# An attention and mixture-of-experts kernel on one core: rows of the negated maxima by VectorE block transposes and ScalarE copies

## What is computed

```python
factor = 2
scale = 1.0 / np.sqrt(D)
q_pool = q.reshape(B, H, S // factor, factor, D).mean(axis=3)
scores = scale * np.matmul(q_pool, k.transpose(0, 1, 3, 2))
scores = scores - np.max(scores, axis=-1, keepdims=True)
attn = np.exp(scores)
attn = attn / (np.sum(attn, axis=-1, keepdims=True) + 1e-09)
return np.matmul(attn, v).astype(np.float32)
```

## Time and profile before

| | us |
|---|---|
| median of 3 runs | 932.74 (932.3 to 933.03) |
| the profiled execution | 933.13 |
| its span, first to last instruction | 931.1 |
| PE busy | 901.1 (97%) |
| DVE busy | 568.9 (61%) |
| ACT busy | 387.7 (42%) |
| POOL busy | 389.2 (42%), all in the attention stage |

### The profile page before, as it was taken

How to read it: one execution, slowest core, us unless ns; L and a number is a source line. 1 busy time by engine, 2 the same in 40 slices (tenths; PEclk the granted TensorE clock), 3 DMA queues, 4 the chain that set the end, 5 groups by cost and what they waited for, 6 DMA issues and landing times.

```text
span 931.1 us, 17697 instructions
## 1 busy us (share of the span) xinstructions
PE 901.1 (97%) x7120; PEld 728.4 (78%) x7120; DVE 568.9 (61%) x966; ACT 387.7 (42%) x740; POOL 389.2 (42%) x269
## 2 busy tenths in 40 slices
PE   4899999999999999999999999999999999999996
PEld 3676766677676766665999999999999999999733
DVE  6988888888888988866554433433443433433423
ACT  3555555565555555555443222322322322322202
POOL 3999999999999989988000000000000000000000
PEclk9999999999999999999999999999999999999999
DMA  6112212222212212303320000200000000377898
GB/s 240 46 59 77 71 36 74 78 78 77 73 57 77 62 43 77 95 1 114 91 91 1 1 1 1 91 1 1 1 1 1 1 1 1 122 239 225 286 382 307
DMA packets 47025, 76.39 MB, mean 82 GB/s; under 512 B 3296, under 2 KB 32608, under 8 KB 46944
## 3 DMA queue, kind: packets, MB, share of 16 engines
q1 hardware_dynamic: 46944, 75.26, 24.2%
HBM read 70.53 MB, written 4.72 MB: 81 GB/s over the span
## 4 chain that ended last, share of the span: by engine, by line
PE 88%; DVE 5%; POOL 2%; DMA 2%; SPq 1%; issue 1%; ACT 1%; POOLq 0%; ACTq 0%
PE psum L611 14%; PE psum L680 8%; PE psum L682 7%; PE psum L664 7%; PE psum L662 7%; PE psum L681 7%; PE psum L663 7%; PE psum L590 6%; PE psum L533 4%; PE psum L593 3%; PE psum L595 3%; PE psum L597 3%; DVE mx L1142 2%; POOL acc L1499 2%; PE psum L493 1%; SPq L469 1%
## 5 line engine op out<-in xcount | busy, mean ns | idle before, releaser
L1499 POOL TENSOR_TENSOR acc<-acc,pt 128x576 f32<-128x576 f32 x220 | 324.1, 1473 | 33.8 <-ACT pt L936 2.8
L936 ACT ACTIVATE pt<-psum 128x576 f32<-128x576 f32 x288 | 174.1, 649 | 121.7 <-PE psum L598 120.6
L1142 DVE TENSOR_REDUCE mx<-psum 128x1 f32<-128x512 f32 x256 | 162.0, 676 | 25.9 <-PE psum L533 25.1
L611 PE MATMUL psum<-pt,vs 128*64 128x288 f32 x1152 | 154.9, 414 | 0.0
L1330 DVE TENSOR_SCALAR gf<-gf 128x384 f32<-128x384 f32 x96 | 34.5, 359 | 196.4 <-ACT gf L1065 196.4
L680 PE MATMUL psum<-gh,W 128*128 128x384 f32 x384 | 133.4, 347 | 0.0
L1065 ACT ACTIVATE gf<-psum 128x384 f32<-128x384 f32 x96 | 47.2, 492 | 200.8 <-PE psum L664 200.2
L681 PE MATMUL psum<-gl,W 128*128 128x384 f32 x384 | 128.5, 335 | 0.0
L682 PE MATMUL psum<-gh,W 128*128 128x384 f32 x384 | 128.4, 334 | 0.0
L664 PE MATMUL psum<-xh,W 128*128 128x384 f32 x384 | 128.4, 334 | 0.0
L662 PE MATMUL psum<-xh,W 128*128 128x384 f32 x384 | 128.4, 334 | 0.0
(11 more groups left out here) (163 smaller groups left out, 1835.5 us busy)
## 6 DMA issues: line engine op xcount, KB each, us to landing
ring<-in_w SPq DMA_DIRECT2D x16, 1024.0 KB, 5.2
ring<-in_w SPq DMA_DIRECT2D x32, 512.0 KB, 7.8
qraw<-in_qT SPq DMA_DIRECT2D x16, 576.0 KB, 4.8
kraw<-in_kT SPq DMA_DIRECT2D x16, 576.0 KB, 3.7
vs<-in_v SPq DMA_DIRECT2D x16, 576.0 KB, 4.0
out<-ob SPq DMA_DIRECT2D x18, 256.0 KB, 4.4
wst<-in_w_in SPq DMA_DIRECT2D x16, 256.0 KB, 2.7
wst<-in_w_out SPq DMA_DIRECT2D x16, 256.0 KB, 3.0
```

Source lines behind the costliest of these rows:

```text
L611: ins = mm(psum[64 * s:64 * s + 64, O_BANK, 0:HALF], vs[:, p % NB, s, kt * D:(kt + 1) * D], pt[:, i % NPT, s, :], start=(kt == 0), stop=(k ...
L936: act.activation(pt[:, i % NPT, :, :], t_pair(("T", h, kt))[:, :, 0:HALF], ACT.Exp, scale=SCALE)\
L1142: dve.tensor_reduce(mx[:, b, u // 2, s, u % 2:u % 2 + 1], bank, AX.X, ALU.max).then_inc(s_red, 1)
L1499: pool.tensor_tensor(a, first, pt[:, i % NPT, :, :], ALU.add).then_inc(s_acc, 1)
```

## The change

PE's transposes of the negated maxima, their three kinds of ring items and ScalarE's copies from PSUM go. `nm2` becomes `nmb` [128, 5 blocks, 2 heads, 32], of which column 0 of each 32 holds the maxima and the rest stays zero, and DVE transposes it in blocks of 32 x 32 to `rows`. There each group of 32 queries (a = 0 to 3 within a block of 128) stands as a row on partition 32a. Copies bring the four partitions' pieces together in `nmT`: one copy for each a and each head, eight a pair, by ScalarE, from one partition to one partition, 5 or 4 blocks of 32 columns each. ScalarE does four after the exponential kt 6 of the odd half and four after kt 8. For pair 0 the first three blocks go by four copies of ScalarE and four of DVE, the others by eight copies of ScalarE after half 0. DVE has three reduces in place of two a pair, then waits for them and transposes. Scores wait for eight copies of a pair. `mx` moves, and the wait for the identity matrix goes to a later user.

```diff
-    r_items = [("S", 0, u) for u in FIRST_UNITS] + [("TRA", 0)]
+    r_items = [("S", 0, u) for u in FIRST_UNITS]
...
-        if h == 0:
-            r_items.append(("TRB", 0))
-        if rows_at(h):
-            r_items.append(("TR", h // 2 + 1))
...
+    def row_to(b, s, a, blocks):
+
+        return nmT[64 * s:64 * s + 1, b, :].rearrange("o (j a c) -> o j a c", a=4, c=32)[:, blocks, a, :]
+
+    def row_from(s, a, blocks):
+        return rows[32 * a:32 * a + 1, blocks, s, :]
+
+    ROW_BLOCKS = (slice(0, 5), slice(0, 5), slice(0, 4), slice(0, 4))
...
-        def max_rows(p):
-            item = ("TR", p)
-            for freed in r_free[item]:
-                pe.wait_ge(*freed)
-            pe.wait_ge(s_nm, 2 * p + 2)
-            lo, hi = r_bank(item, 0), r_bank(item, 1)
-            for j in range(4):
-                nc.tensor.transpose(lo[0:65, j * P:(j + 1) * P], nm2[:, p % 2, j, :], ident[:, :])
-            nc.tensor.transpose(hi[0:65, 0:P], nm2[:, p % 2, 4, :], ident[:, :]).then_inc(s_TR, 1)
...
-                    pe.wait_ge(s_trc, 3 * p + 3)
+                    pe.wait_ge(s_trc, 8 * p + 8)
...
         def read_first_rows():
-            act.wait_ge(s_TRa, 1)
+            act.wait_ge(s_rowsa, 1)
             act.wait_ge(s_zero, 3)
-            act.copy(nmT[0:65, 0, 0:3 * P], r_bank(("TRA", 0))[0:65, 0:3 * P]).then_inc(s_trca, 1)
+            for a in range(4):
+                act.copy(row_to(0, 0, a, slice(0, 3)), row_from(0, a, slice(0, 3))).then_inc(s_trca, 1)
...
-            act.copy(nmT[0:65, b, 0:4 * P], lo[0:65, :]).then_inc(s_trc, 1)
-            act.copy(nmT[0:1, b, 4 * P:SQ], hi[0:1, 0:64]).then_inc(s_trc, 1)
-            act.copy(nmT[64:65, b, 4 * P:SQ], hi[64:65, 64:P]).then_inc(s_trc, 1)
+            for a in range(4):
+                act.copy(row_to(p % 2, s, a, ROW_BLOCKS[a]), row_from(s, a, ROW_BLOCKS[a])).then_inc(s_trc, 1)
...
+                if h % 2 and kt in (6, 8) and p + 1 < NP:
+                    read_rows_of_max(p + 1, (6, 8).index(kt))
...
-            if rows_at(h):
-                read_rows_of_max(p + 1)
...
-            dve.tensor_reduce(nm2[:, b, j:4, 0:65:64], mx[:, b, j:4, :, :], AX.X, ALU.max, negate=True).then_inc(s_nm, 1)
-            dve.tensor_reduce(nm2[:, b, 4, 0:65:64], mx[:, b, 4, 0, :].unsqueeze(1).broadcast_to([P, 2, 3]), AX.X, ALU.max,
-                              negate=True).then_inc(s_nm, 1)
+            dve.tensor_reduce(nmb[:, j:4, :, 0], mx[:, b, j:4, :, :], AX.X, ALU.max, negate=True).then_inc(s_nm, 1)
+            for s in range(2):
+                dve.tensor_reduce(nmb[0:64, 4, s, 0:1], mx[64 * s:64 * s + 64, b, 4, 0, :], AX.X, ALU.max, negate=True)\
+                   .then_inc(s_nm, 1)
+            dve.wait_ge(s_nm, 3 * p + 3)
+            dve.transpose(rows[:, j:5, :, :].rearrange("p j s c -> p (j s c)"),
+                          nmb[:, j:5, :, :].rearrange("p j s c -> p (j s c)")).then_inc(s_rows, 1)
...
+            dve.wait_ge(s_nma, 1)
+            dve.transpose(rows[:, 0:3, :, :].rearrange("p j s c -> p (j s c)"),
+                          nmb[:, 0:3, :, :].rearrange("p j s c -> p (j s c)")).then_inc(s_rowsa, 1)
+            dve.wait_ge(s_rowsa, 1)
+            for a in range(4):
+                dve.tensor_copy(row_to(0, 1, a, slice(0, 3)), row_from(1, a, slice(0, 3))).then_inc(s_trcd, 1)
```

More of the change, by code:

```diff
@@ L94, in soft_moe_kernel @@
                           ("qlr", [P, NB, SQ], F32R))
-    (_, kraw, qs, nmT, pt, vs, acc, khr, qhr, bdq, onesel, nm2, mx, rinv, qraw) = overlay(
+    (_, kraw, qs, nmT, pt, vs, acc, khr, qhr, bdq, onesel, nmb, rows, mx, rinv, qraw) = overlay(
         ("early_weights", [P, W_EARLY * 4 * 512], F32),
@@ L106, in soft_moe_kernel @@
         ("onesel", [P, P], F32R),
-        ("nm2", [P, 2, 5, 65], F32),
+        ("nmb", [P, 5, 2, 32], F32),
+        ("rows", [P, 5, 2, 32], F32),
         ("mx", [P, 2, 5, 2, 3], F32),
@@ L162, in soft_moe_kernel @@
     s_klo, s_qlo, s_klo_first, s_qlo_first = sems("s_klo s_qlo s_klo_first s_qlo_first")
-    s_sum, s_last, s_nma, s_TRa, s_trca = sems("s_sum s_last s_nma s_TRa s_trca")
-    s_Sa, s_Sb, s_Sf, s_red, s_rec, s_nm, s_TR, s_trc = sems("s_Sa s_Sb s_Sf s_red s_rec s_nm s_TR s_trc")
+    s_sum, s_last, s_nma, s_rowsa, s_trca, s_trcd = sems("s_sum s_last s_nma s_rowsa s_trca s_trcd")
+    s_Sa, s_Sb, s_Sf, s_red, s_rec, s_nm, s_rows, s_trc = sems("s_Sa s_Sb s_Sf s_red s_rec s_nm s_rows s_trc")
     s_Ta, s_Tb, s_exp, s_pv, s_acc, s_o = sems("s_Ta s_Tb s_exp s_pv s_acc s_o")
@@ L236, in banks_of @@
     def banks_of(item):
-        return 1 if item[0] in ("SUM", "TRA", "TRB") or item[0] == "S" and item[2] == NU - 1 else 2
+        return 1 if item[0] == "SUM" or item[2] == NU - 1 else 2
     FIRST = 2 * len(FIRST_UNITS)
@@ L256, in soft_moe_kernel @@
                 freed_by[bank] = (s_sum, item[1] + 1)
[L257 to L260, removed]
             else:
@@ L585, in scores @@
             if (h, kt) == (1, 0):
-                pe.wait_ge(s_trc, 3)
+                pe.wait_ge(s_trc, 8)
             lo, hi = (psum[:, k, 0:HALF] for k in t_slot(item))
@@ L904, in read_first_rows, with read_rows_of_max @@
         def read_first_rows():
-            act.wait_ge(s_TRa, 1)
+            act.wait_ge(s_rowsa, 1)
             act.wait_ge(s_zero, 3)
-            act.copy(nmT[0:65, 0, 0:3 * P], r_bank(("TRA", 0))[0:65, 0:3 * P]).then_inc(s_trca, 1)
+            for a in range(4):
+                act.copy(row_to(0, 0, a, slice(0, 3)), row_from(0, a, slice(0, 3))).then_inc(s_trca, 1)
         def read_second_rows():
[L910 to L919, removed]
+            act.wait_ge(s_rows, 1)
+            for s in range(2):
+                for a in range(4):
+                    blocks = slice(3, ROW_BLOCKS[a].stop)
+                    act.copy(row_to(0, s, a, blocks), row_from(s, a, blocks)).then_inc(s_trc, 1)
+        def read_rows_of_max(p, s):
+            act.wait_ge(s_rows, p + 1)
             if p >= 2:
@@ L1156, in negated_max @@
             dve.wait_ge(s_red, max(red_at["S", p, u] + banks_of(("S", p, u)) for u in range(NU)))
-            if p >= 2:
-                dve.wait_ge(s_TR, p - 1)
-            else:
-                dve.wait_ge(s_zero, 3)
+            if p:
+                dve.wait_ge(s_rows, p)
+                dve.wait_ge(s_trc, 8 * p)
             j = 0 if p else 3
-            dve.tensor_reduce(nm2[:, b, j:4, 0:65:64], mx[:, b, j:4, :, :], AX.X, ALU.max, negate=True).then_inc(s_nm, 1)
-            dve.tensor_reduce(nm2[:, b, 4, 0:65:64], mx[:, b, 4, 0, :].unsqueeze(1).broadcast_to([P, 2, 3]), AX.X, ALU.max,
-                              negate=True).then_inc(s_nm, 1)
+            dve.tensor_reduce(nmb[:, j:4, :, 0], mx[:, b, j:4, :, :], AX.X, ALU.max, negate=True).then_inc(s_nm, 1)
+            for s in range(2):
+                dve.tensor_reduce(nmb[0:64, 4, s, 0:1], mx[64 * s:64 * s + 64, b, 4, 0, :], AX.X, ALU.max, negate=True)\
[3 more added lines that the diff above has]
+                          nmb[:, j:5, :, :].rearrange("p j s c -> p (j s c)")).then_inc(s_rows, 1)
         def first_negated_max():
```

42 lines of the change are left out of this document (11 added, 31 removed).

## The result

The changed kernel took 934.67 us (median of 20 runs, 932.72 to 938.67) against 933.36 us for the kernel before in the same comparison: a ratio of 1.0014, interval 1.0008 to 1.0021. It is 1.3 us slower where 4.4 us less were forecast. The profiled execution took 933.52 us, its span is 931.7 us.

What follows compares the result with a forecast made beforehand. PE was taken to bound the attention stage, POOL close behind. Transposes -9.7, ScalarE's copies +4.2 and start +0.7 gave -4.8 us; -4.4 was taken, from the median 932.74 to 928.3 us, 8-in-10 range 925.3 to 934.0.

Steps and rivals of the forecast that it cites:

- pair if the copies cost no more than forecast: Attention pairs: PE's new pair was put at 26.09 - 0.39 = 25.7 us.
- start, to half 2: Start of the attention stage: first blocks' rows, pair 0's copies and pair 1's lost gain sum to +0.7 us.
- two long pairs: Two of fourteen attention pairs ran longer, the longer 26.86 us; counted as still there after the change.
- What leaves PE: Five PE transposes per pair, p = 1 to 15, between scores and products: 0.69 us a pair saved.
- What ScalarE gets: Eight row copies a pair, 1.1 us per group of four, make PE's next scores 0.3 us late; 0.39 gain stays.
- The prediction's own sign of being wrong: Forecast is wrong if mx waits exceed 0.3 us a pair, copies begin over 0.3 apart, or POOL's adds average past 1.5.
- What DVE gets: Per pair one tiny reduce, a wait and a 320-column transpose (0.4 us): 0.6 us in all, overlapping the copies' wait.
- POOL: Next bound in the attention stage: its pair 25.7 to 26.1 us, as good as equal to PE's; 5.0 us idle left.
- rival 3: DVE falls behind at the sum, L1207 waiting within POOL's adds, 0.77 us per affected pair: 936.0 us, chance 0.16.
- the term for the eight copies in a row: Start, after exp 8 of head 0: eight ScalarE copies replace three, 1.0 us more, but only +0.15 with DVE behind anyway.
- Rival 2: Gain used up: copies of 0.31 us or a 0.7 us transpose make PE 0.6 late per pair: 932.1 us, chance 0.18.
- Rival 4: DVE's block transpose takes the port POOL's adds use, +0.35 us per pair for POOL: 932 to 934 us, chance 0.04.

Runs made afterwards that it cites:

- the version with one-input operations: Changed kernel with last unit of maxima and row copies moved earlier, and DVE's remainders of keys and queries (pairs 2 to 15) replaced by one-input operations: 925.46 us, ratio 0.9914.
- a second transpose: Changed kernel with every pair's DVE transpose of 320 columns done twice, once into a tile of its own: 936.78 us, ratio 1.0033.
- The versions whose copies hold nothing up: Changed kernel with second copy group omitted (930.12 us), copies cut to 32 columns (929.32), last maxima unit earlier (931.64), or that plus start's copies spread (931.27).
- the edited start: Changed kernel with pair 0's second rows copied in two groups of four after exponentials kt 6 and 7 of half 0: 934.58 us, again 934.83.
- the version with one transpose: Kernel before the change with one PE transpose of five per pair (p = 1 to 15), nothing new on ScalarE or DVE: 927.61 us, ratio 0.9934.
- DVE's copies: Changed kernel with the second head's four row copies of pairs 1 to 15 on DVE behind its transpose, replacing ScalarE's second group: 986.73 us, ratio 1.0584.
- the version with short copies: Changed kernel with each of the eight row copies of pairs 1 to 15 cut to one block of 32 columns: 929.32 us, ratio 0.9961.

## Why the prediction was wrong, step by step

The forecast's sum for the attention stage was -4.8 us (4.4 was then taken); the dense layer began 2.4 us later. The terms, with their measured sizes:

| step | forecast | measured | difference over 14 pairs |
|---|---|---|---|
| copies hold the first scores, per pair | 0.30 | 0.63, of which 0.31 show in the pair | +4.3 |
| pair if the copies cost no more than forecast | 25.70 | 25.87 (floor by DVE and POOL) | +2.4 |
| start, to half 2 | +0.7 | +2.47 | +1.8 |
| two long pairs, "still there" | 0 | gone | -1.3 |

-4.8 + 4.3 + 2.4 + 1.8 - 1.3 = +2.4. By the medians the kernel is 1.3 us slower, not 2.4; the rest is in the last stages of the two profiles.

*What leaves PE:* nearly right. PE's busy time fell by 0.4 us a pair with 0.5 us of idle time in its place, and the version with one-input operations shows the whole: 25.51 us. That is 0.58 us below the old pair, so the forecast's 0.69 was at least 0.11 too much.

*What ScalarE gets:* the mechanism, its place and its cover were right, and this is the term that failed. The step "by the line between them 160 columns cost 0.28 and 128 columns 0.26" took its slope from a copy of 65 partitions out of PSUM, 0.6 ns a column. The row copies take 323 and 295 ns and follow each other 1.31 us to the group of four, not 1.10; from 32 to 160 columns that is 0.85 ns a column. 0.21 us twice is 0.42, more than the 0.33 by which the wait grew, from 0.30 to 0.63. The prediction's own sign of being wrong, copies beginning over 0.3 us apart, came true at 0.33. The prediction says itself what follows from 0.31 us a copy ("nearly all of the gain"); the likeliest value should have lain between the two.

*What DVE gets:* the transpose of 320 columns took 0.51 us (forecast 0.4; the estimate of 0.78 scaled from the Trainium skill, "VectorE: DVE Perf Modes", section "The three transpose paths", did not come true), one of 192 columns 0.38, one of 128 0.32. That DVE's lateness hides behind the copies' wait was right: a second transpose changed no pair from half 4 on.

*POOL:* right as a bound and wrong as harmless. I had PE's 25.7 and POOL's 25.7 to 26.1 as "as good as equal" and took the smaller. The versions whose copies hold nothing up, four of them, stand at 25.87, 25.88, 25.96 and 25.97. The floor is not POOL alone: PE waits for DVE's reduces there, and the swap of DVE's operations for others brought the pair down to 25.51. It is the loop of DVE and POOL. In both profiles of the changed kernel L1182 fell within an add (1.29 us on average, instead of 0.78 in the earlier trace rows), as rival 3 had it. But the edited start's first profile has it at 0.75 us and a pair at 26.12, so behind the copies' wait rival 3's mechanism cost 0.06 us a pair by these profiles, and not 0.77.

*Start:* the term for the eight copies in a row failed, 0.15 us, "against DVE being behind anyway". PE's scores of half 1 waited for them for 1.39 us and began at 31.78 in place of 30.62, DVE then stood idle for 1.28 us ahead of the reduce at 34.18, and the last reduces of pair 1 began at 43.41 in place of 41.72, 1.69 us later. Up to 0.7 us of that may be the stretch at the lower clock. What comes behind, the transpose and the copies of pair 1, took 0.78 us more than before, as forecast (0.7).

*Rival 2,* "the gain is used up", at 0.18, is what happened, one size further. Rival 4 fell: the transposes took 311 to 515 ns by their size alone whatever POOL did, and POOL's adds did not get longer (1.50 us on average before, 1.48 after). Its mechanism is real for another instruction, the DVE copy.

## What to carry to other kernels

When work leaves the engine that bounds, time the chain that replaces it by the slowest row that fits each new instruction, and count its start-up once per instruction: eight copies of a few hundred nanoseconds in a queue that had 1.4 us of cover made the scores 0.63 us late where at most 0.69 was gained, and left nothing. Then add up what the next engines can do with their waits for each other; here a floor of 25.9 us lay 0.2 us under the old pair of 26.1, so by the length of the pairs freeing PE alone could win about 3 us over fourteen of them (the median of the version with one transpose, 5.8 us lower, is not explained by that). The cure is to make the result earlier rather than cheaper: with the last unit of maxima moved half a pair ahead and the start's copies spread, the same DVE transposes beat both kernels, 931.27 us (ratio 0.9976, 0.9967 to 0.9986), by 2 us or so.

## What the runs showed of the hardware

- A DVE copy on one partition took 0.22 us (96 columns) with POOL idle. With POOL adding, half of the copies of 128 and 160 columns took 0.22 to 0.25 us and most others 1.29 to 1.49, 0.75 us on average; a DVE block transpose took 0.51 us for 320 columns beside the same adds, never more than 0.515.
- A DVE operation with one SBUF input took 0.73 to 0.74 us for 576 columns where the two-input form took 1.80 and 1.96 beside POOL's adds, and 0.75 where it ran outside them.
- PE's waits of 1 to 2 us were followed by 3.4 us at the lower clock level in nearly every pair with DVE's copies (granted clock 0.94 over the five pairs), but a wait of 0.5 us in every pair of the changed kernel never was (1.00). A single wait of that length decided nothing: one of 1.39 us was followed by the lower clock in the changed kernel (at 32.1) and not in the version with short copies.
- Profiles of one kernel differed by 0.7 us at half 1 in when PE's matmuls reached their full speed (0.29 us in place of 0.44 for 288 columns, at 22.1 us in one and after 23.6 in another), and by 2 us at the dense layer.
